# Coarse attention probabilities divided by their sums after the weighing, with sums made by TensorE

## The reference

```
q_d, k_d, v_d = mean over groups of 4 tokens of q, k, v     # 144 groups
a = exp(s - max(s));  a = a / (sum(a) + 1e-9);  out_d = a @ v_d,  s = q_d k_d^T / 8
out_up = repeat(out_d, 4 tokens)                            # coarse attention
mask = |i - j| < 4;  out_local = softmax(masked q k^T / 8) @ v   # band attention
x = (out_up + out_local) as (2304, 512)
h = x @ w_in (512 x 2048);  g = s * relu(h)^2 + b;  x = g @ w_out     # layer 1
h = x @ w2_in;  g = h - tanh(h);  out = g @ w2_out                    # layer 2
```

## Time and profile before

| | us |
|---|---|
| median of 3 runs | 934.83 |
| lowest, highest | 932.21, 936.11 |
| profiled execution | 934.32 |
| its span, first to last instruction | 932.3 |
| TensorE busy | 910.6 (98%) |
| VectorE busy | 496.5 (53%) |
| ScalarE busy | 435.1 (47%) |
| GpSimd busy | 291.4 (31%) |

### The profile page before, as it was taken

The page is one execution under the profiler, slowest core; times in us unless marked ns, Lnnn a source line. Parts: engine busy times, 40 slices in busy tenths (PEclk is TensorE's granted clock), DMA queues, the critical chain, the costliest instruction groups (busy, mean ns, idle before and its releaser), DMA issues.

```text
span 932.3 us, 15655 instructions
## 1 busy us (share of the span) xinstructions
PE 910.6 (98%) x6037; PEld 854.4 (92%) x6037; DVE 496.5 (53%) x647; ACT 435.1 (47%) x1107; POOL 291.4 (31%) x292
## 2 busy tenths in 40 slices
PE   8999989999999999999999999999999999999997
PEld 7889879998999999999999999999999999999996
DVE  4638488989899999992002542422323323322321
ACT  2898666456746674536445742322323223222221
POOL 6567462988478943533222100000000000000000
PEclk8999989999999999999999999999999999999999
DMA  8960552444344322102124500200200200100101
GB/s 220 265 224 12 153 139 56 111 119 102 69 119 105 96 49 46 49 1 94 34 71 137 206 1 1 69 1 1 68 1 1 69 1 1 35 1 0 34 1 35
DMA packets 48239, 65.16 MB, mean 70 GB/s; under 512 B 18151, under 2 KB 29989, under 8 KB 48165
## 3 DMA queue, kind: packets, MB, share of 16 engines
q1 hardware_dynamic: 46916, 62.59, 24.4%
q10 hardware_dynamic: 1248, 1.57, 0.6%
HBM read 54.71 MB, written 9.44 MB: 69 GB/s over the span
## 4 chain that ended last, share of the span: by engine, by line
PE 76%; DVE 6%; ACT 5%; POOL 4%; SPq 3%; DMA 3%; issue 3%; DVEq 0%; ACTq 0%; POOLq 0%
PE acc L1821 21%; PE hid L1803 21%; PE acc L1784 15%; PE hid L1764 15%; POOL own L949 2%; DVE prod L1130 1%; PE pa L1728 1%; DMA wa_raw<-in_moe_w_in_dram 1%; POOL xl L963 1%; DMA own<-in_k_dram 1%; PE pa L1700 1%; SPq L809 1%; ACT pc L1408 1%; DVE sc L1139 1%; DVE prod L1215 1%
## 5 line engine op out<-in xcount | busy, mean ns | idle before, releaser
L972 POOL TENSOR_TENSOR gl<-relu,gh 128x288 fp32r<-128x288 f32 x128 | 122.7, 960 | 194.4 <-PE acc L1784 147.8
L1784 PE MATMUL acc<-gh,wbh 128*128 128x288 f32 (+1 forms) x512 | 155.6, 304 | 0.0
L1764 PE MATMUL hid<-xh,wah 128*128 128x288 f32 x512 | 155.3, 305 | 0.0
L1784 PE MATMUL acc<-gl,wbh 128*128 128x288 f32 (+1 forms) x512 | 151.5, 296 | 0.0
L1784 PE MATMUL acc<-gh,wbl 128*128 128x288 f32 (+1 forms) x512 | 151.2, 295 | 0.0
L1764 PE MATMUL hid<-xh,wal 128*128 128x288 f32 x512 | 151.1, 296 | 0.0
L1269 DVE TENSOR_TENSOR gdif<-hid,tanh 128x384 f32<-128x384 f32 x96 | 53.5, 557 | 183.0 <-ACT tanh L1534 183.0
L1764 PE MATMUL hid<-xl,wah 128*128 128x288 f32 x512 | 148.2, 296 | 2.3 <-POOL xl L963 2.3
L1534 ACT ACTIVATE tanh<-hid 128x384 f32<-128x384 f32 x96 | 47.1, 491 | 187.2 <-PE hid L1803 187.2
L1803 PE MATMUL hid<-x2h,wah 128*128 128x384 f32 x384 | 129.0, 336 | 0.3 <-DVE gdif L1269 0.3
L1803 PE MATMUL hid<-x2h,wal 128*128 128x384 f32 x384 | 129.0, 336 | 0.0
(11 more groups left out here) (146 smaller groups left out, 1579.4 us busy)
## 6 DMA issues: line engine op xcount, KB each, us to landing
wa_raw<-in_moe_w_in_dram SPq DMA_DIRECT2D x8, 1024.0 KB, 7.5
wb_raw<-in_moe_w_out_dram SPq DMA_DIRECT2D x8, 1024.0 KB, 6.5
kl<-in_k_dram SPq DMA_DIRECT2D x23, 240.0 KB
vl<-in_v_dram SPq DMA_DIRECT2D x23, 240.0 KB
x2T<-ystage SPq DMA_DIRECT2D x8, 576.0 KB, 3.2
x2raw<-x2T SPq DMA_DIRECT2D x6, 768.0 KB, 4.5
own<-in_q_dram SPq DMA_DIRECT2D x11, 384.0 KB
own<-in_k_dram SPq DMA_DIRECT2D x9, 384.0 KB
```

Source lines behind the costliest of these rows:

```text
L972: g.tensor_tensor(out=gl[:, turn % LRING1, 0:NS], in0=relu[:, f % 2, :], in1=gh[:, turn % GRING1, 0:NS].bitcast(F32), op=ALU.subtract).the ...
L1764: one = pe.matmul(dst, w[:, d, cols], x[:, j % XRING, d, :], start=i == 0, stop=i == len(products) - 1)
L1784: one = pe.matmul(acc[:, d, n], w[:, f, cols], g[:, turn % ring, n], start=(f == 0 and p == 0), stop=(f == FT - 1 and p == 2))
```

## The change

In a score step the sums are no longer accumulated, and `score_inverse` and `score_scale` are gone: the exponentials are transposed as they are. The grouped values `vd` get 64 columns of the number 4.0 between the two heads of a pair, so that each weighing matmul has 128 output columns: the weighted values of its head on one half of the partitions, and four times the sum of its probabilities on the other. A new step `sum_up` (ScalarE) copies the sums to `up`, across to the partitions of the values, and adds 4e-9. `place_up` goes to VectorE: a reciprocal in place, and two multiplications with the values out of PSUM. It frees the bank.

The first four weighings of b 0 no longer go through `pa` but to the free columns of `hid`'s banks, behind the band attention's output of the same head pair. The low parts of x of tile 0 are made by VectorE. The rounding of the first weight blocks follows `dense_place(2)`, the later ones follow `x_high(0, 3)`, where they followed `place_up(0, 3)` or nothing. `dense_add` has a lower rank. Three score buffers in place of four, some merged small tensors, and steps that no configuration used (`w1_rest`, `minus`) are taken out.

```diff
-SCORES = 4
+SCORES = 3
+def in_opening(b, n):
+    return b == 0 and n < NPAIR
...
-        if turn > 1:
-            after.append(("place_up", 0, NPAIR - 1))
+        if turn > 2:
+            after.append(("x_high", 0, KT - 1))
+        else:
+            after.append(("dense_place", 2))
...
-        o.add("DVE", 0.55, (0, 0, 0), ("dense_add", a), [("dense_values", a), ("place_up", 0, a)])
+        o.add("DVE", 0.55, (0, 0, 8), ("dense_add", a), [("dense_values", a), ("place_up", 0, a)])
...
-            o.add("ACT", 1.0, (0 if b else -1, b, 6 + 2 * i), ("score_exp", b, i), after, empties=("scores", b, i))
-            o.add("DVE", 0.2, (0, b, i), ("score_inverse", b, i), [("score_exp", b, i)], .8 if b else 0.6)
-            o.add("ACT", 0.64, (0 if b else -1, b, 7 + 2 * i), ("score_scale", b, i), [("score_inverse", b, i)])
-            after = [("score_scale", b, i)]
+            o.add("ACT", 0.6, (0 if b else -1, b, 6 + 2 * i), ("score_exp", b, i), after, empties=("scores", b, i))
+            after = [("score_exp", b, i)]
...
-                o.add("ACT", 0.22, (0 if b else -1, b, 9 + 2 * i), ("place_up", b, w), [("weigh", b, w)], empties=("weigh", b, w))
+                opening = in_opening(b, w)
+                if opening:
+                    after += [[("dense_keys", 3)], [("dense_queries", 3)], [("dense_add", 0)], [("dense_add", 1)]][w]
+                o.add("PE", 0.4, (0, b, 8 + 2 * i), ("weigh", b, w), after, lead(b, qh), fills=not opening)
+                o.add("ACT", 0.5 if b else 0.4, (0 if b else -1, b, 9 + 2 * i), ("sum_up", b, w),
+                      [("weigh", b, w)] + ([("dense_values", w)] if opening else []))
+                o.add("DVE", 0.9 if b else 0.65, (0, 0, 8) if opening else (0, b, i), ("place_up", b, w), [("sum_up", b, w)], .8 if b else 0.3,
+                      empties=None if opening else ("weigh", b, w))
...
+            if j == 0:
+                o.add("DVE", 0.5, (0, 0, 9), ("x_low", j, d), [("x_high", j, d)])
+            else:
+                o.add("POOL", pool(NS), (0,), ("x_low", j, d), [("x_high", j, d)])
...
-    vd, _ = place("vd", [P, 2, HEADS, HD], F32)
+    vd, _ = place("vd", [P, 2, NPAIR, 3, HD], F32)
+    def weighed(b, n):
+        hp, cols, count = upper(b, n)
+        width = cols.stop - cols.start
+        if in_opening(b, n):
+            return hid[:, n % 2, NS:NS + 2 * width], s_dweigh, n + 1
+        r, m = bank("weigh", b, n)
+        return pa[:, r, 0:2 * width], s_full[r], m
+        ve.memset(vd[:, :, :, 1, :], float(GROUP)).then_inc(s_vones, 1)
...
+            elif kind == "place_up":
+                ve.wait_ge(s_usum, 2 * count)
+                ve.reciprocal(up[:, hp, cols], up[:, hp, cols]).then_inc(done, 1)
+                ve.wait_ge(done, before + 1)
+                for h2 in range(2):
+                    rows = slice(h2 * HD, (h2 + 1) * HD)
+                    ve.tensor_tensor(up[rows, hp, cols], src[rows, h2 * width:(h2 + 1) * width], up[rows, hp, cols],
+                                     ALU.mult).then_inc(emptied if h2 else done, 1)
...
+            elif kind == "sum_up":
+                sc.wait_ge(there, filled)
+                if in_opening(b, n):
+                    sc.wait_ge(s_dout, n + 1)
+                for h2 in range(2):
+                    rows, others = slice(h2 * HD, (h2 + 1) * HD), slice((1 - h2) * HD, (2 - h2) * HD)
+                    sc.activation(up[rows, hp, cols], src[others, h2 * width:(h2 + 1) * width], ACT.Copy,
+                                  bias=GROUP * 1e-9).then_inc(s_usum, 1)
...
-                        one = pe.matmul(pa[h2 * HD:(h2 + 1) * HD, r, 0:cols.stop - cols.start],
-                                        vd[0:HG, kh, 2 * hp + h2, :], pT[0:HG, h2, kh, cols],
+                        one = pe.matmul(dst[:, h2 * width:(h2 + 1) * width],
+                                        vd[0:HG, kh, hp, h2:h2 + 2, :].rearrange("p t d -> p (t d)"),
+                                        pT[0:HG, h2, kh, cols],
                                         start=kh == 0, stop=kh == 1)
```

More of the change, by code:

```diff
@@ L215, in plan @@
             after.append(("dense_values", NPAIR - 1))
-        if turn > 1:
-            after.append(("place_up", 0, NPAIR - 1))
+        if turn > 2:
+            after.append(("x_high", 0, KT - 1))
+        else:
+            after.append(("dense_place", 2))
         o.add("ACT", act(512), (2, turn) if turn > 2 else (1, 0, 5), ("w1_high", f, half), after)
         maker = low_maker(f, half)
[L220 to L224, removed]
+        if maker == "DVE":
             o.add("DVE", add(512), (0, 0, 24), ("w1_low", f, half), [("w1_high", f, half), ("dense_add", NPAIR - 1)])
@@ L732, in build @@
     low_of = {}
-    for engine in ("POOL", "DVE", "ACT"):
+    for engine in ("POOL", "DVE"):
         for n, step in enumerate(one for one in o.order[engine] if one[0] == "w1_low"):
@@ L739, in wait_low, with upper @@
         count = low_of["w1_low", f, half]
[L740 to L744, removed]
-    high_of = {step: n + 1 for n, step in enumerate(one for one in o.order["ACT"] if one[0] == "w1_high")}
+        e.wait_ge(s_w1vlow if maker == "DVE" else s_w1low, count)
+    high_of = {step: n + 1 for n, step in enumerate(one for one in o.order["ACT"] if one[0] == "w1_high")}
+    def upper(b, n):
+        if b == 0:
+            hp, qh = score_of(b, n)
+            return hp, slice(qh * HG, (qh + 1) * HG), n + 1
+        return n, slice(0, GROUPS), weighs(0) + weighs(1) * (b - 1) + n + 1
+    def weighed(b, n):
[5 more added lines that the diff above has]
+        return pa[:, r, 0:2 * width], s_full[r], m
     def dense_out(a):
@@ L1366, in scalar_program @@
                               ).then_inc(s_w1high, 1)
-            elif kind == "w1_low":
-                f, half = key
-                r, m = bank("w1_rest", f, half)
-                sc.wait_ge(s_full[r], m)
-                sc.activation(half_of(f, half, wal, wbl), pa[:, r, :] if half else
-                              pa[:, r, :].rearrange("p (k n) -> p k n", k=KT), ACT.Copy).then_inc(s_free[r], 1)
             elif kind == "place_columns":
@@ L1431, in scalar_program @@
                     if i > 1:
[L1432 to L1433 removed]
+                        src, there, filled = weighed(b, i - 2)
+                        sc.wait_ge(there, filled)
                 else:
@@ L1441, in scalar_program @@
                               ).then_inc(s_free[r], 1)
-            elif kind == "place_up":
+            elif kind == "sum_up":
                 b, n = key
-                r, m = bank("weigh", b, n)
+                hp, cols, count = upper(b, n)
+                src, there, filled = weighed(b, n)
+                width = cols.stop - cols.start
                 if b > 1 and n == 0:
@@ L1576, in tensor_program @@
                 one.then_inc(s_full[r], 1)
-            elif kind == "w1_rest":
-                f, half = key
-                r = room(kind, *key)
-                pe.wait_ge(s_minus, 1)
-                pe.wait_ge(s_w1high, high_of["w1_high", f, half])
-                pe.matmul(pa[:, r, :], ident[:, :], half_of(f, half, wa_raw, wb_raw), start=True, stop=False)
-                pe.matmul(pa[:, r, :], minus[:, :], half_of(f, half, wah, wbh), start=False, stop=True
-                          ).then_inc(s_full[r], 1)
             elif kind == "dense_turn":
@@ L1719, in tensor_program @@
                     n, (2 * n, 2 * n + 1), slice(0, GROUPS))
+                width = cols.stop - cols.start
+                pe.wait_ge(s_vones, 1)
                 wait_sums(pe, b, 7 + 2 * hp)
```

106 lines of the change are left out of this document (47 added, 59 removed).

## The result

The changed kernel takes 939.22 us (median of 9 runs, 937.34 to 941.21), the kernel before 933.69 us (9 runs beside them, 931.93 to 936.53). The ratio is 1.0057, with a 95% interval of 1.0041 to 1.0073: slower, where the forecast was 2.1 us faster. The sign is settled: the interval lies wholly above 1, and the ratio a little above the half per cent that the prediction took as the limit of what can be told. (In microseconds 939.22 still falls inside the band from 930.2 to 939.5 that the prediction called the same, since the kernel before was 1.1 us quicker beside it than in its first three runs.)

A forecast was written before the change was run, and what follows sets the result against it. TensorE, 98% busy, bounds, with the opening and tiles 1 and 2 deciding. From 934.32 us: -4.3 opening, -2.0 late chain, +0.7 VectorE, +1.0 and +2.0 weighing, +0.5 banks = -2.1, so 932.2 us; range 925.5 to 941.

The forecast's parts named there:

- The weighing: TensorE's weighing matmuls with 128 output columns: +1.0 us for b 0 and 1, +2.0 us for b 2 and 3.
- The opening: Stretch up to the end of hidden1(0,0): ends at 45.6 us in place of 49.9, -4.3 us; bounds 1.9 to 7.1 gained.
- The four weighings lie between fillers there and cost nothing: Opening, on TensorE: the four weighings there add no time; x_high no longer waits behind weight roundings.
- what is late: Opening: VectorE is late next, one step after the other from 29.58 us to the normalization's end at 38.58.
- best bound of 42.8 us: Opening's earliest end: dense_norm ending at 37.2, no contention, place_up at 0.6 us; 7.1 us gained.
- The late chain: b 0's late score steps (50 to 70 us) pass the banks sooner with less ScalarE latency: -2.0 us, at most 4.
- below nothing: Lower bound of the weighing's price: the 0.19 us behind each weighing goes, twelve times 0.12 us.
- VectorE in the stream: VectorE's sixteen place_up: +0.7 us at tile 2 (bounds 0 to 5), +0.5 for banks freed later (0 to 8).
- The opening is hidden anyway: Rival, chance 0.10: hidden1 starts 4 us earlier, but the stop at 120 us grows by 4; 937.5 us.
- VectorE becomes the bound: Rival, chance 0.22: from 117 us on, +5.0 at tile 2 and +7 for banks held; 942 us.
- TensorE's idle time from 190 to 340 us: Sign for the forecast: TensorE idle about 3 us in that stretch.
- wrong if the opening ends after 48: Sign against the forecast: the opening, put at 45.6 us, ends later than 48 us.

The follow-up runs named there:

- both: The changed kernel with 64 output columns per weighing matmul (sums left out) and layer 2's tensors at the old place; 1.0003 of the kernel before, 935.77 us.
- x2_back: The changed kernel with layer 2's tensors in the attention's space 128 bytes higher, where the kernel before has them; 1.0028 of the kernel before, 936.63 us.
- x2_down: The kernel before with small tensors merged and layer 2's tensors where the change has them, 128 bytes lower; 1.0032 of the kernel before, 936.85 us.
- split_x: The kernel before with x2h and x2l 128 bytes higher and x2raw, tanh, gdif and ostage 256 higher; 1.0022 of the kernel before.
- rec2_opening: The changed kernel with reciprocals of the opening's four place_up over 2 columns in place of 72; 1.0052 of the kernel before.
- late_first: Two runs, tile 2's first key_products following late_add(3) in place of late_values(3): 1.012 in the changed kernel, 1.0039 in the kernel before.
- w64: The changed kernel with 64 output columns per weighing matmul, sums left out, same instructions behind; 1.0027 of the kernel before, 936.93 us.
- rec2_stream: The changed kernel with every place_up reciprocal outside the opening over 2 columns in place of 72 or 144; 1.0056 of the kernel before.
- x2_p256: The kernel before with all layer 2 tensors in the attention's space moved up by 256 bytes; 1.0003 of the kernel before.
- split_rest: The kernel before with x2raw, tanh, gdif and ostage 128 bytes higher, x2h and x2l unmoved; 0.999 of the kernel before.
- x2_p128: The kernel before with layer 2's tensors in the attention's space 192 bytes higher, 128 past a multiple of 256; 1.005 of the kernel before.

## Why the prediction was wrong

Apart from the weighing, the prediction summed the change to -5.1 us (-4.3 opening, -2.0 late chain, +0.7 and +0.5 for VectorE). The run both, without the wide weighing and the moved tensors, shows 1.0003, which is +0.3 us with 1.4 of doubt. The step that failed is this one: gains of the opening and of the late chain were carried to the end of the kernel in full, and they are not. Beside it a term of +2.6 us, layer 2, stood at nothing. The weighing was forecast at +3.0 and measured at 2.8.

**Not in the sum at all: layer 2, +2.6 us.** The prediction has no term for the merged small tensors. Taking their shift out (x2_back, 2.7 us by the ratios), putting it in (x2_down, 3.0 us) and moving `x2h` and `x2l` alone (split_x) show it. This term by itself turns -2.1 into about +0.5.

**The opening: 1.8 us in place of 4.3 (the bound given was 1.9).** Over more profiles it is 2.1: hidden1(0,0) ends at 48.1 us in the mean of seven with the change's opening and at 50.2 in that of eight with the old one, and takes 1.84 us for 3.46 (the two with 64 output columns take 2.57). Two claims failed. "The four weighings lie between fillers there and cost nothing": the first of 1.08 us stood ahead of the scores, for which VectorE waited 1.10 us at 35.82, and dense_norm(3) ended at 39.1, not 37.7; the third and fourth (2.00 us at 41.40) stood ahead of dense_values(3). And VectorE was not what is late throughout: rec2_opening takes its reciprocals away, and hidden1(0,0) still starts right behind TensorE's fillers. TensorE's and VectorE's queues hold each other there. The sizes on VectorE were right: a `place_up` is 0.59 + 0.49 us. (The best bound of 42.8 us leaves out the 0.4 us for the last matmul that the estimate has; with it the bound is 43.2, and 6.7 us gained.)

**The late chain: -2.0 forecast.** The step read the 2.31 us stop as the end of a chain that a quicker ScalarE would shorten. It is an order on VectorE, `late_add` behind a `key_products` of 2.49 us, and it became 2.81 us. Tile 0 did get shorter, 75.77 to 74.26 us. Five of seven profiles with the order of before have 75.3 to 75.8 us there (the other two 77.4), and six with that of the change 73.8 to 75.9, 74.8 in the mean: about 0.7 us shorter, so a part of the 2.0 may be there, and whether ScalarE brought it is open. What both shows is that time won ahead of tile 2 is not kept: tiles 2 to 6 are 2.8 us longer. That VectorE sets the pace there fits the stops behind its steps and late_first, but no run separates it from the order in which the planner laid the steps.

**The weighing: mechanism right, and the size too.** It takes 0.98 us for 144 columns against 0.96. For 72 columns it takes 0.81 to 0.92 us up to the start of what follows (1.08 and 1.01 in the timeline include the modelled end of the last matmul), against 0.9. That half the columns save so little is seen in the spacing: an instruction follows the one before after 0.11 us with 72 columns and 0.12 us with 144. The gain behind (0.19 us) is there. +3.0 was forecast; width 64 gives 2.8 back by the ratios and about 3.2 by the rows. The prediction put the gain of 0.19 both into its range of 0.1 to 0.3 and at "below nothing"; the true net is 0.14 to 0.20 for 144 columns and about 0.3 for 72. The Trainium skill ("TensorEngine Tiling (Array Packing)", Key Properties) has both halves, tiles that work in parallel and a drain at a change of mode; w64 agrees, with 0.33 us saved and 0.19 paid.

**VectorE in the stream: +0.7 and +0.5.** TensorE's idle time in tiles 0 to 6 is 10.3 us for 9.9, so +0.3 as a sum, near the forecast by luck: tile 0 has 1.9 less, and tiles 2 to 6 have 6.4 for 4.4. rec2_stream has 5.8 there, so the load of the reciprocals is at most 0.6 of these 2.0. The stops stand where a maximum or an addition comes behind a long band product, which speaks for the order; the two multiplications of each `place_up` were in no run taken away. (For b 1 eight inverses of 154 ns are 1.2 us less work, not the 0.8 of the prediction, which changes little.)

**The rivals.** "The opening is hidden anyway" (937.5, chance 0.10) came nearest, in time and in what tiles 0 to 6 did: both's 1.0003 says that the opening's gain is given back in full, though in tiles 2 to 6 rather than at 120 us. That its 937.5 is only 1.7 us off is in part luck, for it has no term for layer 2 either. "VectorE becomes the bound" (942, 0.22) did not happen as it was put: TensorE's table of waits names no `place_up`, and tile 2 started 1.5 us sooner. Of the signs named, the reciprocals, the weighing and the product behind came as written; TensorE's idle time from 190 to 340 us was 5.3 us, where "about 3" was named (it is 3.2 in the kernel before); "wrong if the opening ends after 48" came true by 0.06 us. The range held the time, but the forecast was on the wrong side of the time before.

## What to carry to other kernels

A merged or moved tensor is a change: compare the addresses of everything that TensorE streams, and compare the pace of stages that nothing edited before explaining those that were. A stop that ends behind a long instruction on the releasing engine is an order, and where the engine behind it is 94% busy, as here, neither a sooner start nor a removed stop was worth its length. Price a matmul with few moving columns from a row of that shape: here 72 columns in place of 144 made the eight instructions of a weighing only some 0.07 us shorter.

## What the hardware showed that was not expected

The pace of fp32 matmuls of 384 columns depends on where in SBUF their moving operand starts: twelve take 2.08 us at 192 bytes modulo 256, 2.11 at 0 and at 128, and 2.12 at 64, and split_x moved no operand of TensorE but that one. Over 96 steps that is up to 0.4% of this kernel, and 0.5% with the output steps at 128.

And two runs of one order of work can differ by 2 us in tile 0, as x2_p256 (77.35 us) and split_rest (75.32) do, with one stop of 2.6 or 0.6 us for VectorE's sums of a freshly loaded tensor. The two sums themselves take longer, first x2_p256, then split_rest:

```profile
108.73 1.06 DVE L1150 TENSOR_TENSOR own<-own 128x384 f32<-128x384 f32 x1 [2.69 <-DMA own<-in_k_dram]
109.82 1.99 DVE L1153 TENSOR_TENSOR ks<-own 128x192 f32<-128x192 f32 x1
```

```profile
109.12 0.56 DVE L1151 TENSOR_TENSOR own<-own 128x384 f32<-128x384 f32 x1 [2.80 <-DMA own<-in_k_dram]
109.71 0.36 DVE L1154 TENSOR_TENSOR ks<-own 128x192 f32<-128x192 f32 x1
```

What differs is which of two loads landed first. In x2_p256 and x2_p128 GpSimd starts its own row of sums and subtractions 0.1 to 0.2 us ahead of VectorE's, and VectorE's two take 3.1 and 3.0 us with it. In the six other profiles with that order of work up to there GpSimd starts 0.3 to 0.6 us behind, and they take 0.9 to 1.5 us. Why VectorE is slower beside GpSimd is not shown here; it fits the multiplication that took 1.43 us beside GpSimd's work and 0.50 alone.
